# Shorter steps between a search and its expert, another share of filling, and narrower counting matmuls

## The chip, the cores and the metric

The kernel runs on 1 core of a Trainium2 chip. The metric is the time of one execution on the device in microseconds (us), the median of several runs. A profiled execution gives the rows below; its times count from the start of its span.

## The reference

Three layers in a row, on 4 sequences of 768 positions (3072 tokens of 512 features), all float32.

1. Banded attention, 8 heads of 64: each query sees the keys less than 16 positions away and the maxima of all 24 blocks of 32 keys (with the block means as values).
2. A first expert layer. The logits x @ w_gate of all tokens and 8 experts are sorted, and tokens are assigned greedily until an expert has CAP = 384 tokens. Then relu(x @ w1[e]) @ w2[e] for the tokens of each expert:

```
    for idx in order:
        tok, e = (int(idx) // E, int(idx) % E)
        if assigned[tok] >= 0 or counts[e] >= cap:
            continue
        assigned[tok] = e
```

3. A second expert layer with a skip score: out = x, and where x @ w_skip > 0, plus the gate weight times the chosen expert's two products.

## The kernel before

The work is written out by hand for each engine, and semaphores tie the engines together. It has four parts.

**Opening and attention.** 16 units (a sequence and a pair of heads), each of three groups of windows. SyncE's queue issues all loads in order. VectorE clears the borders of the key tiles `kc` and the gaps of `qz`, then the padded gates `wg1` and `wg2` (L941, L942), and signals `pads_ready`; TensorE runs seven matmuls on the padding as filling (L1404), then the scores of the first group (L1339, L1342). Behind attention, tiles of 128 token rows of its output are transposed on TensorE (`x_rows_tile`, L1399), copied out by ScalarE (L748) through four buffers and stored (L378). A buffer is written again only when its store has landed.

**Searches.** The greedy assignment closes one expert at a time, in 8 searches (`search(ph)` on VectorE, `window(w)` on TensorE). In each, V holds every token's best logit among the experts still open. It is transposed (L1547, L1548) into Vt, and 17 rounds look for the threshold bit by bit: VectorE counts how many values reach up to three candidates (L1028), TensorE adds the counts over partitions (CNT, L1557), VectorE picks the next candidates (L1043, L1045). A matmul spreads the threshold of each expert (TAU, L1567); VectorE takes the largest, `tau`, and the expert that has it (`oneE`, `e_f`, `e_i`). `e_i` lets SyncE load that expert's weights W1 and W2, 2 MB each (L381, L385). Then VectorE marks the tokens above `tau` and at it (GT), adds them up along the row (`scn`), and copies the row totals to `rowt` (L1072). Two matmuls turn these into offsets (BAS and BASN, L1571, L1572), and VectorE computes each token's `slot` (L1083). From that come one-hot tiles (`hot` L1092, `hot_blk` L1094, `hot_id` L314 and L315: on VectorE in search 0, on GpSimd in the others). TensorE folds them into a list (L1503), VectorE copies it (`folded`, L1000), TensorE unfolds it (L1511), and VectorE writes the token numbers `gidx` (L1006). GpSimd then gathers the rows of the expert's tokens in three tiles (L593), counted by one semaphore `xg_in`. Meanwhile VectorE takes the closed expert and the taken tokens out of the logits LM (L1099 to L1103) and forms the next V (L988 to L1015); the copies of `folded` and `gidx` stand between these steps.

**Products between the counts.** TensorE's list is fixed when the program is written. Expert k needs 3 transposes of rows (L1468), 32 products of the first layer (`product_1`, two instructions of 384 columns, L1479), 24 of the second (`product_2`, two instructions of 512 columns, L1493), and a tail for the second layer's gate. Each of these has a number of units: 3 for a first-layer product, 4 for a second-layer one, 2 for a transpose of rows. `room(w)` gives how many units may be placed in each of 22 gaps of window w: one before the rounds, 17 behind the counts, and four behind TAU, BAS, the fold and the lists. An item is placed when the running sum of units allows it whole. Window w carries the products of expert w - 1; window 0 has none, and TensorE runs filling matmuls there (`keep_busy`, L1540), as in the first two rounds of window 1. What is left runs behind search 7. TensorE keeps the order of its list: a wait holds all that stands behind it.

**Second layer.** Tiles of 128 tokens through layer1 (L1608) and layer2 (L1626), 4 MB of weights for each.

The count matmul reads `cnt` (8 columns) sixteen times over, so it has 128 columns; TAU, BAS and BASN have 128 columns too, of which 8, 2 and 1 are read.

## Time and profile before

| | |
|---|---|
| median of 3 runs | 844.89 us (843.51 to 848.12) |
| profiled execution | 842.21 us |
| its span | 840.4 us |
| TensorE matmuls busy | 800.1 us (95%) |
| VectorE busy | 465.7 us (55%) |
| ScalarE busy | 228.4 us (27%) |
| GpSimd busy | 216.2 us (26%) |

Attention ends at about 144 us of the span, search 0 at 194; the first product of the first expert layer starts at 203.60, and the last search's lists are read at about 544. From some 607 on the second layer runs. The 95% is a mean over stages: it does not say that TensorE is the limit in each. Matmuls are pipelined and the ends are modelled, so the distance from one start to the next says more than a busy time.

### The profile page before, as it was taken

To read this page: it belongs to the slowest core of one execution; us is meant where nothing else is said; L and a number is where in the kernel's file an instruction comes from. 1 tells how busy PE (TensorE), PEld (TensorE's weight loads), DVE (VectorE), ACT (ScalarE), POOL (GpSimd) and SP (SyncE) were. 2 spreads that over 40 slices of the span, in tenths; PEclk is the share of its full clock that TensorE was granted. 3 is DMA by queue.
4 is the path that set the end of the run, shared out by engine and by line. 5 is a ranking of instruction groups with operands and counts; after the bars stand their busy time and mean duration, and the time that the engine had idled before them with its cause. 6 is when DMAs were issued, how large, how long until landed. Compare 5 with 4: busy or idle time off the path is not lost.

```text
span 840.4 us, 15143 instructions
## 1 busy us (share of the span) xinstructions
PE 800.1 (95%) x5002; PEld 512.0 (61%) x5002; DVE 465.7 (55%) x2153; ACT 228.4 (27%) x681; POOL 216.2 (26%) x313
## 2 busy tenths in 40 slices
PE   7999998897899999999999999999999999999996
PEld 6878786785445455454544545455577686777762
DVE  7989896777777676776766677507049100000000
ACT  6888786501103121120211212121111111110101
POOL 7888883001030120302112030120300321111110
PEclk9999999999999999999999999999999999999999
DMA  9967650625070531706225071436988999898983
GB/s 272 294 226 220 205 144 21 266 69 186 0 284 30 190 123 25 264 25 236 77 102 186 26 265 48 166 147 257 356 313 312 414 350 346 309 344 305 331 322 114
DMA packets 64505, 171.66 MB, mean 204 GB/s; under 512 B 5584, under 2 KB 5584, under 8 KB 64448
## 3 DMA queue, kind: packets, MB, share of 16 engines
q1 hardware_dynamic: 54512, 143.70, 48.5%
q0 software_dynamic: 6480, 20.91, 6.9%
q10 hardware_dynamic: 3456, 6.29, 1.9%
q8 instruction: 36, 0.59, 0.3%
q14 instruction: 21, 0.17, 0.1%
HBM read 148.41 MB, written 22.81 MB: 204 GB/s over the span
## 4 chain that ended last, share of the span: by engine, by line
PE 74%; DVE 13%; DMA 5%; issue 3%; POOL 2%; SPq 1%; ACT 1%; DVEq 0%; POOLq 0%; ACTq 0%
PE bank L1493 17%; PE bank L1479 16%; PE bank L1626 11%; PE bank L1608 11%; DVE junk L1028 5%; PE bank L1342 3%; PE bank L1369 3%; PE bank L1351 2%; DMA kc<-in_kT 2%; PE bank L1557 2%; DMA weights<-in_moe_w 1%; PE bank L1468 1%; PE bank L1684 1%; PE bank L1339 1%; PE bank L1652 1%
## 5 line engine op out<-in xcount | busy, mean ns | idle before, releaser
L1479 PE MATMUL bank<-features,weights 128*128 128x384 f32 x512 | 182.3, 497 | 0.6 <-ACT features L753 0.6
L1493 PE MATMUL bank<-weights 128*128 128x512 f32 x384 | 179.2, 602 | 0.0
L1028 DVE TENSOR_SCALAR_CACHE_REDUCE junk<-Vt,cand 128x192 bf16<-128x192 f32 x376 | 136.1, 409 | 4.8
L1479 PEld LDWEIGHTS bank<-features,weights 128*128 128x128 f32 x512 | 89.5, 191 | 50.6 <-issue 5.6
L1608 PEld LDWEIGHTS bank<-x2T,weights 128*128 128x128 f32 x896 | 102.2, 192 | 5.9 <-issue 5.9
L1608 PE MATMUL bank<-x2T,weights 128*128 128x128 f32 x896 | 102.6, 275 | 0.0
L1493 PEld LDWEIGHTS bank<-weights 128*128 128x128 f32 x384 | 66.8, 190 | 58.4 <-issue 56.5
L1626 PE MATMUL bank<-weights,h2T 128*128 128x512 f32 x224 | 98.8, 593 | 0.4 <-ACT h2T L820 0.4
L1188 DVE SCALAR_TENSOR_TENSOR o<-bank,gate,x 128x512 f32<-128x512 f32 x14 | 10.5, 751 | 155.0 <-PE bank L1626 155.0
L758 ACT ACTIVATE weights<-bank 128x384 f32<-128x384 f32 x64 | 31.4, 491 | 141.3 <-PE bank L1479 141.3
L1626 PEld LDWEIGHTS bank<-weights,h2T 128*128 128x128 f32 x224 | 41.3, 190 | 46.5 <-issue 46.5
L702 ACT ACTIVATE pr<-bank,nmx 128x120 f32<-128x120 f32 x192 | 67.0, 374 | 5.1 <-DVE nmx L899 4.9
L820 ACT ACTIVATE h2T<-bank 128x512 f32<-128x512 f32 x28 | 16.6, 597 | 161.9 <-PE bank L1608 161.9
L314 POOL TENSOR_TENSOR hot_id<-hot,pnum 128x384 bf16<-128x384 f32 x7 | 8.2, 1168 | 180.2 <-DVE hot L1092 180.2
L1342 PEld LDWEIGHTS bank<-kw,qz 128*128 128x128 f32 x384 | 51.5, 195 | 1.0
L503 POOL TENSOR_TENSOR pr<-pr,rinv 128x480 f32<-128x480 f32 x48 | 47.3, 986 | 15.7 <-DVE rinv L905 14.1
L1342 PE MATMUL bank<-kw,qz 128*128 128x120 f32 x384 | 51.2, 277 | 0.0
L1043 DVE TENSOR_SCALAR_CACHE_REDUCE reached<-bank 128x7 f32<-128x7 f32 x120 | 19.9, 166 | 54.5 <-PE bank L1557 54.5
L762 ACT ACTIVATE weights<-bank 128x512 f32<-128x512 f32 x24 | 14.3, 598 | 126.9 <-PE bank L1493 126.9
L1557 PEld LDWEIGHTS bank<-cnt,same_e 128*128 128x128 bf16 x136 | 13.1, 96 | 57.2 <-DVE junk L1028 53.7
L593 POOL DMA_INDIRECT weights<-x_rows,gidx x24 | 23.6, 985 | 89.6 <-DVE gidx L1006 59.5
L600 POOL DMA_INDIRECT out<-weights,tok_i x24 | 23.7, 986 | 85.1 <-ACT weights L762 82.2
(333 smaller groups left out, 1056.7 us busy)
## 6 DMA issues: line engine op xcount, KB each, us to landing
weights<-in_moe_w SPq DMA_DIRECT2D x52, 2048.0 KB, 9.9
vw<-in_vwin SPq DMA_DIRECT2D x16, 576.0 KB, 5.1
qc<-in_qT SPq DMA_DIRECT2D x16, 384.0 KB, 5.6
kc<-in_kT SPq DMA_DIRECT2D x16, 384.0 KB, 6.1
vc<-in_vT SPq DMA_DIRECT2D x16, 384.0 KB, 7.4
x_rows<-xr SPq DMA_DIRECT2D x24, 256.0 KB, 2.3
y_rows<-weights ACTq DMA_DIRECT2D x24, 256.0 KB, 2.0
weights<-x_rows,gidx POOLq DMA_INDIRECT x24, 3.7
```

Of the source, the lines that this page charges most:

```text
L503: g.tensor_tensor(pr[:, n % NP, :, :], pr[:, n % NP, :, :], rinv[:, n % NP, :].unsqueeze(2).to_broadcast([128, GW, KW]), ALU.mult) \
L600: g.indirect_dma_start(out=out, out_offset=bass.IndirectOffsetOnAxis(ap=tok_i[:, j:j + 1], axis=0), in_=yb[:, j, :], in_offset=None).then_ ...
L702: ins = a.activation(pr[:, n % NP, w, :], SC[n % 3][:, KW * w:KW * w + KW], ACT.Exp, scale=SCALE, bias=nmx[:, n % NP, w:w + 1], accum_out= ...
L758: a.activation(hT[:, r, :], HB[r % 2][:, 0:CAP], ACT.Relu).then_inc(s["h_act"], 1)
L1028: ins = ve.tensor_scalar(junk[:, c, :], Vt[:, :], cand[:, c:c + 1].bitcast(fp32), 0.0, ALU.is_ge, ALU.add, accum_out=cnt[:, c:c + 1])
L1342: ins = mm(SC[n % 3][:, KW * w:KW * w + KW], qz[u % 2][:, GW * gr + w, :], kw[u % 2][:, GW * gr + w, :], start=False, stop=(w == GW - 1))
L1369: ins = mm(OB[n % 2][D * j:D * j + D, QW * w:QW * w + QW], vw[i][:, GW * gr + w, D * j:D * j + D], pT[:, n % 2, 128 * w + QW * j:128 * w + ...
L1479: ins = mm(HB[r % 2][:, 0:CAP], w1[:, c, 128 * r:128 * r + 128], xgT[:, c, :], start=(c == 0), stop=(c == KC - 1))
L1493: ins = mm(YB[j % 2][:, :], hT[:, r, 128 * j:128 * j + 128], w2[:, r, :], start=(r == 0), stop=(r == FC - 1))
L1557: mm(CNT, same_e[:, :], cnt[:, :].unsqueeze(1).to_broadcast([128, WIDE // 8, 8]), start=True, stop=True).then_inc(s["cnt_mm"], 1)
L1608: ins = mm(HB2[h][:, 128 * c:128 * c + 128], W1[:, buf, k * F + at:k * F + at + 128], x2T[par][:, k, :], start=(k == 0), stop=(k == KC - 1))
L1626: ins = mm(YB2[par][:, :], h2T[:, f, :], W2[:, buf, f * DM:f * DM + DM], start=(f == 0), stop=(f == FC - 1))
```

## The change

In VectorE's chain behind the threshold, comparisons and products are joined in one instruction, the expert number is computed behind the row totals, and the two base matmuls add up in PSUM, so that their result is read as a pointer scalar without copies. `oneE` is finished later, ahead of the update of LM. In search 0's list `folded` and `gidx` are copied earlier (`first_list`). CNT, TAU and BAS become as narrow as what is read. The gathered tiles have a semaphore each, and TensorE, SyncE and GpSimd wait for these; on GpSimd and SyncE all three are waited for where `xg_in` was. Two row tiles instead of four stand ahead of window 0, the others move two later. `room()` changes for windows 1 and 2, and the filling changes in window 0, in the first rounds of window 1, and at the opening, where the gate padding is cleared first.

```diff
-    WIDE = 128
...
-        diag = sb("diag", [E, WIDE])
+        diag = sb("diag", [E, E])
...
-        rowt = sb("rowt", [128, WIDE], bf16)
-        base = sb("base", [128, 4])
+        rowt = sb("rowt", [128, 3], bf16)
+        rank = sb("rank", [128, 2, NT])
...
-        VTP, CNT, TAU = SM[:, 0:256], SM[:, 256:256 + WIDE], SM[:, 384:384 + WIDE]
-        BAS, BASN, FOLD, IDS = SM[:, 0:WIDE], SM[:, WIDE:2 * WIDE], SM[0:2 * SB, 384:384 + SLOTS // SB], SM[:, 448:448 + CT]
+        VTP, CNT, TAU = SM[:, 0:256], SM[:, 256:264], SM[:, 384:384 + E]
+        BAS, FOLD, IDS = SM[:, 0:2], SM[0:2 * SB, 384:384 + SLOTS // SB], SM[:, 448:448 + CT]
...
-                        .then_inc(s["xg_in"], 16)
+                        .then_inc(s[f"xg_in{j}"], 16)
...
+            ve.memset(wg1[:, :, :], 0.0)
+            ve.memset(wg2[:, :, :], 0.0).then_inc(s["pads_ready"], 1)
             for i in range(NB):
                 ve.memset(kc[i][:, 0:BAND], 0.0)
...
-            ve.memset(wg1[:, :, :], 0.0)
-            ve.memset(wg2[:, :, :], 0.0).then_inc(s["pads_ready"], 1)
             block_maxima(0)
...
                 o.step(ve.tensor_reduce(m, src, X, ALU.max))
+                first_list = isinstance(ids_of, int) and ids_of == 0
+                if first_list:
+                    fold_out(ids_of)
                 o.step(ve.tensor_tensor(tmp, src, bc(m, shape, 2), ALU.is_equal))
-                if ids_of is not None:
+                if first_list:
+                    ids_out(ids_of)
+                elif ids_of is not None:
                     fold_out(ids_of)
...
-                if ids_of is not None:
+                if ids_of is not None and not first_list:
                     ids_out(ids_of)
...
-                o.step(ve.tensor_reduce(tau[:, :], TAU[:, 0:E], X, ALU.max))
-                o.step(ve.tensor_scalar(oneE[:, :], TAU[:, 0:E], tau[:, :], None, ALU.is_equal))
-                o.step(ve.tensor_tensor(oneE[:, :], oneE[:, :], revE[:, :], ALU.mult))
+                o.step(ve.tensor_reduce(tau[:, :], TAU, X, ALU.max))
+                o.step(ve.scalar_tensor_tensor(out=oneE[:, :], in0=TAU, scalar=tau[:, :], in1=revE[:, :],
+                                               op0=ALU.is_equal, op1=ALU.mult))
                 o.step(ve.tensor_reduce(oneM[:, :], oneE[:, :], X, ALU.max))
-                o.step(ve.tensor_scalar(oneE[:, :], oneE[:, :], oneM[:, :], None, ALU.is_equal))
+                o.step(ve.scalar_tensor_tensor(out=t1[:, :, :], in0=bc(oneE[:, :], full, 1), scalar=oneM[:, :], in1=V[:, :, :],
+                                               op0=ALU.is_equal, op1=ALU.mult))
+                o.step(ve.tensor_reduce(mx[:, :], t1[:, :, :], X, ALU.add))
+
+                o.step(ve.tensor_scalar(GT[:, 0, :], mx[:, :], tau[:, :], None, ALU.is_gt))
+                o.step(ve.tensor_scalar(GT[:, 1, :], mx[:, :], tau[:, :], None, ALU.is_equal))
+                for h in range(2):
+                    o.step(ve.tensor_tensor_scan(scn[:, h, :], GT[:, h, :], zero1[:, :], 0.0, ALU.add, ALU.add))
+                ve.tensor_copy(rowt[:, 1:3], scn[:, :, NT - 1]).then_inc(s["rows_ready"], 1)
+                o.step(ve.scalar_tensor_tensor(out=rank[:, :, :], in0=scn[:, :, :], scalar=float(-BIG_SLOT), in1=GT[:, :, :],
+                                               op0=ALU.add, op1=ALU.subtract))
                 o.step(ve.tensor_scalar(e_f[:, :], oneM[:, :], -1.0, float(E), ALU.mult, ALU.add))
                 if not isinstance(ph, int) or ph > 0:
                     dve.wait_ge(s["expert_read"], ph)
                 ve.tensor_copy(e_i[:, :], e_f[:, :]).then_inc(s["expert_ready"], 1)
-                o.step(ve.tensor_tensor(t1[:, :, :], V[:, :, :], bc(oneE[:, :], full, 1), ALU.mult))
...
-                dve.wait_ge(s["base_mm"], ph + 1)
-                o.step(ve.tensor_copy(base[:, 0:2], BAS[:, 0:2]))
-                o.step(ve.tensor_copy(base[:, 2:3], BASN[:, 0:1]))
-                o.step(ve.tensor_tensor(base[:, 1:2], base[:, 1:2], base[:, 2:3], ALU.add))
+                dve.wait_ge(s["base_mm"], ph + 1)
                 for h in range(2):
-
-                    o.step(ve.scalar_tensor_tensor(out=scn[:, h, :], in0=scn[:, h, :], scalar=base[:, h:h + 1],
-                                                   in1=GT[:, h, :], op0=ALU.add, op1=ALU.subtract))
-                    o.step(ve.scalar_tensor_tensor(out=scn[:, h, :], in0=scn[:, h, :], scalar=float(-BIG_SLOT),
+                    o.step(ve.scalar_tensor_tensor(out=rank[:, h, :], in0=rank[:, h, :], scalar=BAS[:, h:h + 1],
                                                    in1=GT[:, h, :], op0=ALU.add, op1=ALU.mult))
...
                 o.step(ve.tensor_scalar(sel[:, :], slot[:, :], CAP - 0.5, None, ALU.is_lt))
-
+                o.step(ve.tensor_scalar(oneE[:, :], oneE[:, :], oneM[:, :], None, ALU.is_equal))
...
-            for _ in range(7):
+            for _ in range(11):
                 mm(LG[0:32, 0:128], wg2[:, 0, :], wg2[:, :, :].rearrange("p c e -> p (c e)"), start=True, stop=True)
...
-            for t in range(4):
+            for t in range(2):
                 x_rows_tile(t)
...
                 if w == 1:
-                    return [0] + [0, 0, 6] + [6] * (ROUNDS - 3) + [15, 28, 4, 8]
-                return [8] + [9, 8] * 7 + [9] * 3 + [15, 28, 4, 4 if w == 2 else 8]
+                    return [0] + [0, 6] + [6, 9, 6, 6] * 3 + [6, 9, 6] + [13, 22, 4, 8]
+                if w == 2:
+                    return [8] + [9, 8] * 7 + [8] * 3 + [13, 22, 4, 4]
+                return [8] + [9, 8] * 7 + [9] * 3 + [15, 28, 4, 8]

             def load_x(k, j):
-                if j == 0:
-                    pe.wait_ge(s["xg_in"], 16 * CT * (k + 1))
-
+                pe.wait_ge(s[f"xg_in{j}"], 16 * (k + 1))
...
-                keep_busy(w, 3)
+                keep_busy(w, 4)
...
                 if w == 0:
-                    x_rows_tile(4)
-                    x_rows_tile(5)
+                    x_rows_tile(2)
+                    x_rows_tile(3)
+                if w == 1:
+                    keep_busy(0, 5)
                 keep_busy(w, 2)
...
-                    mm(CNT, same_e[:, :], cnt[:, :].unsqueeze(1).to_broadcast([128, WIDE // 8, 8]),
-                       start=True, stop=True).then_inc(s["cnt_mm"], 1)
-                    if w == 0 and n < NT // 2 - 3:
-                        x_rows_tile(2 * n + 6)
-                        x_rows_tile(2 * n + 7)
-                    keep_busy(w, 3 if n < NT // 2 - 3 else 6)
-                    if w == 1 and n < 2:
-                        keep_busy(0, 6)
+                    mm(CNT, same_e[:, :], cnt[:, :], start=True, stop=True).then_inc(s["cnt_mm"], 1)
+                    if w == 0 and n < NT // 2 - 2:
+                        x_rows_tile(2 * n + 4)
+                        x_rows_tile(2 * n + 5)
+                    keep_busy(w, 3 if n < NT // 2 - 2 else 6)
+                    if w == 1 and n == 0:
+                        keep_busy(0, 7)
...
-                keep_busy(w, 14)
+                keep_busy(w, 11)
...
-                mm(BAS, tri[:, :], rowt[:, :], start=True, stop=True)
-                mm(BASN, ones_bf[:, :], rowt[:, :], start=True, stop=True).then_inc(s["base_mm"], 1)
-                keep_busy(w, 22)
+                mm(BAS, tri[:, :], rowt[:, 1:3], start=True, stop=False)
+                mm(BAS, ones_bf[:, :], rowt[:, 0:2], start=False, stop=True).then_inc(s["base_mm"], 1)
+                keep_busy(w, 17)
...
-                keep_busy(w, 2)
+                keep_busy(w, 1)
                 ids(w)
-                keep_busy(w, 5)
+                keep_busy(w, 9)
```

## Rows read from the trace of the kernel before

**Rows 1.** Busy time by stretch: busy us (instructions) of each engine, granted clock, DMA share, GB/s.

```profile
196.00:252.00 56.00, 49.40 (x199) 24.60 (x200) 40.98 (x238) 6.81 (x13) 8.85 (x11) 1.00 0.45 157
...
302.45:353.04 50.59, 50.02 (x218) 25.72 (x217) 35.91 (x204) 9.61 (x19) 8.40 (x11) 1.00 0.36 130
```

**Rows 2.** Chain of waits in the opening: start us, us, what.

```profile
9.02 15.14 DMA kc<-in_kT
```

**Rows 3.** Timeline of the opening: start, us, engine, line, operation, count, [idle before it].

```profile
3.23 3.20 PE L1404 MATMUL bank<-wg 128*32 128x128 f32 x14 [3.23 <-DVE wg L942]
...
7.05 1.90 PE L1342 MATMUL bank<-kw,qz 128*128 128x120 f32 x8
...
9.47 1.05 PE L1342 MATMUL bank<-kw,qz 128*128 128x120 f32 x8
```

**Rows 4.** Timeline around the start of search 0 and its fifteenth count.

```profile
145.77 0.21 DVE L934 TENSOR_TENSOR V<-LM,t 128x48 f32<-128x48 f32 x1
...
146.85 0.27 PE L1547 MATMUL bank<-ident,V 128*128 128x128 f32 x1
...
150.54 0.65 PE L1399 MATMUL bank<-ident,xT 128*128 128x128 f32 x4 [1.17 <-ACT xr L748]
...
153.59 0.23 PE L1557 MATMUL bank<-cnt,same_e 128*128 128x128 bf16 x1
...
176.45 0.23 PE L1557 MATMUL bank<-cnt,same_e 128*128 128x128 bf16 x1 [0.28 <-DVE junk L1028]
```

**Rows 5.** Two matmul lines: duration ns min/median/max, first and last start, form.

```profile
L1557 PE MATMUL bank<-cnt,same_e x136: 219/219/230, 148.7 to 530.3; 128*128 128x128 bf16 x136
...
L1511 PE MATMUL bank<-folded,unfold x64: 161/162/174, 192.5 to 544.4; 32*128 32x3 bf16 x64
```

**Rows 6.** Timeline of VectorE in the tail of search 0.

```profile
181.88 0.17 DVE L1056 TENSOR_REDUCE tau<-bank 128x1 f32<-128x8 f32 x1 [1.20 <-PE bank L1567]
...
185.06 0.17 DVE L1072 CAST rowt<-scn 128x2 bf16<-128x2 f32 x1
...
187.18 0.18 DVE L1083 SCALAR_TENSOR_TENSOR slot<-scn 128x24 f32<-128x24 f32 x1
...
193.48 0.16 DVE L1006 CAST gidx<-bank 128x3 int32<-128x3 f32 x1
```

**Rows 7.** Chain of waits up to the first product.

```profile
196.83 4.04 DMA weights<-x_rows,gidx
...
202.26 0.67 PE bank L1468 x4
...
203.60 0.59 PE bank L1479
```

**Rows 8.** Timeline, the queue of SyncE: the first expert's weights.

```profile
184.42 0.43 SPq L381 DMA_DIRECT2D weights<-in_moe_w  x1
```

**Rows 9.** Timeline of TensorE in the tail of search 2.

```profile
279.49 0.48 PE L1567 MATMUL bank<-diag,ones 8*128 8x128 f32 x2
279.91 2.85 PE L1479 MATMUL bank<-features,weights 128*128 128x384 f32 x8
283.43 0.23 PE L1571 MATMUL bank<-rowt,tri 128*128 128x128 bf16 x1 [0.67 <-DVE rowt L1072]
...
283.55 6.23 PE L1493 MATMUL bank<-weights 128*128 128x512 f32 x14
289.71 0.77 PE L1503 MATMUL bank<-hot_blk,hot_id 128*32 128x24 bf16 x24
...
293.45 0.33 PE L1547 MATMUL bank<-ident,V 128*128 128x128 f32 x1 [0.58 <-DVE V L1015]
```

**Rows 10.** Timeline of TensorE in search 3.

```profile
323.87 0.23 PE L1557 MATMUL bank<-cnt,same_e 128*128 128x128 bf16 x1 [0.24 <-DVE junk L1028]
323.93 2.15 PE L1479 MATMUL bank<-features,weights 128*128 128x384 f32 x6
325.92 0.22 PE L1557 MATMUL bank<-cnt,same_e 128*128 128x128 bf16 x1
```

More of the change, by code:

```diff
@@ L262, in banded_attention_two_moe_layers @@
             onehot_ready blk_ready id_mm idp_ready ids_ready tok_c
[L263 removed]
+            xg_in0 xg_in1 xg_in2 xg_tr xgT_ready w_in0 w_in1 w_in2 w_in3 w2_in0 w2_in1 w2_in2 w2_in3 w1_lanes w2_lanes h_mm h_act y_mm y_evac y_tr yT_ready l2_mm l2T_ready l2_tr l2_evac y_out y_st y_written
             gate_sub gate_exp rows8_ready base8_mm teA_ready onehot2_ready id2_mm gid2_ready route2_ready
@@ L383, in load_weights @@
                 if rows_first:
-                    sp.wait_ge(s["xg_in"], 16 * CT)
+                    for j in range(CT):
+                        sp.wait_ge(s[f"xg_in{j}"], 16)
                 sp.dma_start(W2[:, 2 * par, :].rearrange("p (c f) -> p c f", c=FC),
@@ L612, in _ @@
             keep_ids(0)
-            pool.wait_ge(s["xg_in"], 16 * CT)
+            for j in range(CT):
+                pool.wait_ge(s[f"xg_in{j}"], 16)
             with pool.Fori(1, E) as ph:
@@ L619, in _ @@
                 keep_ids(ph)
-                wait(pool, "xg_in", 16 * CT * (ph + 1))
+                for j in range(CT):
+                    wait(pool, f"xg_in{j}", 16 * (ph + 1))
                 o.leave(E)
@@ L1071, in search @@
                     o.step(ve.tensor_tensor_scan(scn[:, h, :], GT[:, h, :], zero1[:, :], 0.0, ALU.add, ALU.add))
-                ve.tensor_copy(rowt[:, 0:2], scn[:, :, NT - 1]).then_inc(s["rows_ready"], 1)
+                ve.tensor_copy(rowt[:, 1:3], scn[:, :, NT - 1]).then_inc(s["rows_ready"], 1)
+                o.step(ve.scalar_tensor_tensor(out=rank[:, :, :], in0=scn[:, :, :], scalar=float(-BIG_SLOT), in1=GT[:, :, :],
+                                               op0=ALU.add, op1=ALU.subtract))
+                o.step(ve.tensor_scalar(e_f[:, :], oneM[:, :], -1.0, float(E), ALU.mult, ALU.add))
+                if not isinstance(ph, int) or ph > 0:
+                    dve.wait_ge(s["expert_read"], ph)
+                ve.tensor_copy(e_i[:, :], e_f[:, :]).then_inc(s["expert_ready"], 1)
                 dve.wait_ge(s["base_mm"], ph + 1)
-                o.step(ve.tensor_copy(base[:, 0:2], BAS[:, 0:2]))
-                o.step(ve.tensor_copy(base[:, 2:3], BASN[:, 0:1]))
-                o.step(ve.tensor_tensor(base[:, 1:2], base[:, 1:2], base[:, 2:3], ALU.add))
                 for h in range(2):
-                    o.step(ve.scalar_tensor_tensor(out=scn[:, h, :], in0=scn[:, h, :], scalar=base[:, h:h + 1],
-                                                   in1=GT[:, h, :], op0=ALU.add, op1=ALU.subtract))
-                    o.step(ve.scalar_tensor_tensor(out=scn[:, h, :], in0=scn[:, h, :], scalar=float(-BIG_SLOT),
+                    o.step(ve.scalar_tensor_tensor(out=rank[:, h, :], in0=rank[:, h, :], scalar=BAS[:, h:h + 1],
                                                    in1=GT[:, h, :], op0=ALU.add, op1=ALU.mult))
-                o.step(ve.scalar_tensor_tensor(out=slot[:, :], in0=scn[:, 0, :], scalar=float(BIG_SLOT),
-                                               in1=scn[:, 1, :], op0=ALU.add, op1=ALU.add))
+                o.step(ve.scalar_tensor_tensor(out=slot[:, :], in0=rank[:, 0, :], scalar=float(BIG_SLOT),
+                                               in1=rank[:, 1, :], op0=ALU.add, op1=ALU.add))
                 if not isinstance(ph, int) or ph > 0:
```

7 lines of the change are left out of this document (1 added, 6 removed).

## The prediction

> **What bounds the kernel now.** I read the busy times by stretch first. From the third search on, TensorE is busy for 50.02 of 50.59 us, in six stretches alike, at a granted clock of 1.00: there an edit pays only if it shortens TensorE's own list or an idle gap. In the stretch that holds search 1 it is busy for 49.40 of 56.00 us [rows 1]; search 0, ahead of it, has no product to cover it at all. The chain of waits is read next: in the opening it hangs on a load of kc that takes 15.14 us and lands at 24.16 [rows 2]. The timelines then show, for search 0, a chain that alternates between VectorE and one small matmul [rows 4, 6], the row gather behind it [rows 7], and in the later windows which instruction ends a gap [rows 9, 10].
>
> I sum against the profiled execution, 842.21 us (span 840.4 and 1.8 around it). The median of the runs is 844.89, 2.7 above it; I subtract the same gain from the median.
>
> **Opening.** The padding memsets go ahead of the other memsets, so filling starts some 1.8 us earlier (before: at 3.23) with 22 matmuls instead of 14. The eight score matmuls that started at 7.05 took 1.90 us, the next eight 1.05 [rows 3]: the first were still at the lower of TensorE's two clock levels, 1.2 GHz, and the earlier filling may save up to 0.9 there. I count 0: the kc load behind it was issued by a queue that never waited, and its landing [rows 2] holds VectorE's next maxima whatever TensorE does. Bounds: -0.3 (zeros written later) to 0.9.
>
> **Search 0, up to the last count.** V is done at 145.98, but its transposes start at 146.85, since tiles 2 and 3 and the filling stand ahead [rows 4]. With two tiles and four fills ahead, TensorE is free at about 145.6 and starts at 146.05: 0.8 sooner. Then tile 7 waited 1.17 us for ScalarE [rows 4], which waited for the stores of the first tiles; the third count came at 153.59. The stores land as before, but tiles run two later in the list: tile 6 goes at 150.5, tile 7 at 151.15, its six fills end at 152.25, and the third count starts at 152.3, 1.3 sooner (0.8 of them the start, 0.5 the smaller stall). From there a round takes 22.86/12 = 1.905 us [rows 4], VectorE's turn. A count matmul lasts 219 ns with 128 columns and one with 3 columns lasts 162 [rows 5]: 0.45 ns a column, so 8 columns give 165, and 0.053 less a round. Thirteen rounds: 0.7. The threshold matmul comes 2.0 sooner; itself it goes from 128 to 8 columns in two passes, each 0.107 less streaming: 0.2. VectorE starts on tau 2.2 sooner.
>
> **Search 0, from tau to the first product.** From tau to the row totals took 3.18 us (181.88 to 185.06) [rows 6]. Two narrow steps merge or go, and e_f and e_i move behind: four steps at about 0.18, as narrow ones last there; the wide step takes a pointer scalar (+0.07, bound 0 to 0.15): 0.64 less. From totals to slot took 2.12 us [rows 6]: two copies, an add and two steps of the four before the last go; rank, e_f and e_i run while TensorE sums, and the totals land at about +0.5, rank and its followers end at +0.55. Two pointer steps of 0.27 follow: 1.1 in all, 1.0 less. From slot to gidx took 6.30; oneE now adds 0.26, but the fold is copied one step and gidx three steps sooner (0.39 each, less 0.15 of waiting for the second matmul group): 0.7 less. gidx comes 2.2 + 0.64 + 1.0 + 0.7 = 4.5 us sooner, at 189.0. V of search 1, which pays oneE and the wait, comes 3.3 sooner (190.95 for 194.2).
> The third gather thus lands at 196.4 for 200.87. Before, TensorE then took two transposes, a wait for ScalarE and a third, 2.73 us to the first product [rows 7]; with a semaphore for each tile only the third is left, 202.26 to 203.60 in the same chain, 1.35. The product can start at 197.8 for 203.6. The weights don't stop it: e_i moves behind 1.7 us of other work, so they are issued at 184.0 for 184.42 [rows 8], and 8.0 us to landing gives 192.
>
> **Window 1.** Unit counts from room() and the list give the items per round; a first-layer product costs 1.99/3 = 0.665 [rows 10], a second-layer one 6.16/7 = 0.88 [rows 9], a count 0.055. Rows go in round 1 instead of 2, and its third transpose waits for the gather (196.45), so the third count is at 197.0; products start behind it. Four of the later rounds hold three products (2.05 us), nine hold two (VectorE's 1.85). The last count falls at 223.7 for 227.1: 3.4 sooner, with 18 units (4.0 us) more done. Behind it stands one second-layer product instead of two first-layer ones, 0.45 less ahead of the threshold. TensorE's gap ahead of the row totals in this tail and in that of search 2 (0.67 there [rows 9]) shrinks by 0.6. At the transposes for search 2 the kernel is 5.6 us early and 10 units (2.6 us) ahead in work: 8.2 gained.
>
> **Window 2.** It carries 2.6 us less work, so that lead is spent on time. Its tail is planned too short: from row totals to transposes TensorE has 7.2 us of items for a chain that took 10.0 (283.43 to 293.45, with 0.58 idle [rows 9]) and will take 9.3. That is 1.0 more idle than before; four short rounds add 0.2, the row-total gap gives back 0.85, the threshold 0.2: 0.2 lost.
>
> **Windows 3 to 7.** Their allowances are unchanged, but the sum up to search 2 is 349 units for 350, so whole items fall differently: four rounds instead of two hold only 1.31 to 1.33 us of work. Such a round costs what VectorE needs: 0.24 idle is shown, 1.805 - 1.365 = 0.44 from start to start [rows 10]; after, 0.39. The tally gives 1.81 us of idle in the rounds for 0.95. Against it go the gaps at totals, fold, lists and transposes, 0.5, and the threshold and base matmuls, 0.24: the first took 0.42 from its start to the next [rows 9] and becomes about 0.2. Net 0.1 lost a window, 0.8 with the change of phase. Nothing behind search 7 moves by itself.
>
> **Does a narrow count free TensorE?** Ahead of the next product 0.06 us passed after a 128-column count [rows 10]. I leave it: the next weights are 128 columns of f32 and load behind it. The other bound is the fold, 24 columns with narrow weights: (0.77 - 0.17)/23 = 0.026 [rows 9]. Between 0.055 and 0.026 I take the first, the row of this very pair.
> The Trainium skill (TensorE: Matmul & The Clock Gate, "Back-to-back issue gap") puts matmuls of 1 to 64 columns at a floor near 25 ns; by it the counts would shrink so, and the second rival would be the forecast.
>
> Sum: 8.2 - 0.2 - 0.8 = 7.2 us; my round-by-round tally, which puts the old windows at 50.08 for 50.59, gives 7.1. 842.21 - 7.1 = 835.1 profiled, 844.9 - 7.1 = 837.8 as the median.
>
> **Rivals.**
> Narrow counts pay on TensorE: 0.029 in some 95 counts that stand between products, 2.7 more, 835.1. For it: the fold's pace; against: its weights are 32 columns of bf16.
> The gain is partly given back in the steady windows: the items shifted between rounds include transposes that wait on ScalarE. Each further 0.5 a window costs 2.5, gain 4.6, 840.3. For it: two more short rounds are certain; against: order within the list is the same.
> The gather wait takes the place of the mended chain: the row transposes now stand a round earlier, ahead of count 2, so a late gather holds the search in full. If the gathers, issued from 189.5, queue behind the weights until 192 and lose 4 us, the gain is 3.1, 841.8. Against: the weights' traffic ends about a microsecond before their landing.
> Slower: TensorE's clock. The 128-column counts were padding; narrower, with two tiles less ahead, they could let the level fall to 1.2 GHz in the rounds of search 0 or window 1. A round with six fills then takes 2.7 for 1.85, one with two products 2.77: 0.9 each. From the eighth such round the gain of 7.1 is gone; fifteen rounds cost 13.5, giving 851.3. Against: in window 1 the rounds were no denser than 1.39 of 1.905, and the clock stood at 1.00 [rows 1].
> The Trainium skill (same page, "The HAM clock gate") has the clock follow how busy TensorE was lately; that speaks for this rival, and the trace bears it out only in the opening.
>
> **How the numbers follow.** Forecast 0.66 (own range 835 to 841, from the bounds above and the runs' scatter), narrow counts pay 0.10, given back 0.12, gather 0.07, clock 0.05. A measurement tells about 0.5% from no change, 4.2 us, so faster means below 840.7. Nearly all of the forecast, all of the narrow counts, half of the third and a third of the fourth case: 0.79 faster; 0.16 within; the clock 0.05 slower. Range 833.5 to 842.5: it takes in four cases.
>
> **What would show it.** Right: the first transposes of V near 146.05; rounds of 1.85 in search 0; tau to row totals 2.5 and totals to slot 1.1; the first product near 197.8; short rounds four a window from search 3 on, with periods of 50.5 to 50.9; kc still on the chain at 24. Wrong: a period below 50.2 (narrow counts pay), a level of 0.50 in the slices, a gap ahead of the third count of window 1 of more than 0.6, or a start of V's chain that has moved with the opening.

## The result, and the profile after

The changed kernel takes 839.61 us (median of 6 runs, 838.37 to 841.90) beside 846.29 for the kernel before on the same chip: a ratio of 0.9938 with a 95% interval of 0.9913 to 0.9963. It is faster by 0.6%, 5.2 us on the 844.89 shown; the interval reaches from 3.1 to 7.4 us. (The quotient of the two medians is 0.9921, inside this interval.) Forecast were 7.1 us less (837.8, range 833.5 to 842.5): right within its range, with a size missed by 1.9 us, which the interval alone would not tell from a hit; the trace below shows where it was lost. The profiled execution took 839.7 us, its span 837.9.

The chain of waits (start, us, what) still hangs on kc in the opening, and it landed later than before [rows 2], at 25.94 for 24.16:

```profile
10.03 15.91 DMA kc<-in_kT
```

All that follows has this 1.8 us on it: attention ends at 145.69 for 143.90. Below, "from attention" counts from the first transpose of a row tile behind attention (L1402), which takes that difference out. Of the timeline (start, us, engine, line, what, count, [idle before it]) these are the lines of search 0 and its tail that answer to [rows 4, 6, 7]:

```profile
145.69 1.04 PE L1402 MATMUL bank<-ident,xT 128*128 128x128 f32 x8
...
147.91 0.33 PE L1550 MATMUL bank<-ident,V 128*128 128x128 f32 x1 [0.28 <-DVEq L1018]
...
153.43 0.18 PE L1562 MATMUL bank<-cnt,same_e 128*128 128x8 bf16 x1
...
167.82 0.66 PE L1402 MATMUL bank<-ident,xT 128*128 128x128 f32 x4 [0.72 <-ACT xr L750]
...
181.68 0.17 DVE L1063 TENSOR_REDUCE tau<-bank 128x1 f32<-128x8 f32 x1 [1.15 <-PE bank L1571]
...
184.21 0.17 DVE L1075 CAST rowt<-scn 128x2 bf16<-128x2 f32 x1
...
185.33 0.18 DVE L1086 SCALAR_TENSOR_TENSOR slot<-rank 128x24 f32<-128x24 f32 x1
...
190.95 0.16 DVE L1013 CAST gidx<-bank 128x3 int32<-128x3 f32 x1 [0.26 <-PE bank L1514]
...
198.24 0.63 PE L1471 MATMUL bank<-ident,weights 128*128 128x128 f32 x4 [0.34 <-ACT features L755]
...
199.56 1.56 PE L1482 MATMUL bank<-features,weights 128*128 128x384 f32 x4 [0.68 <-ACT features L755]
```

Tau to row totals is 2.53 us (3.18 before), totals to slot 1.12 (2.12), slot to gidx 5.62 (6.30). The first product is 53.87 us behind the end of attention, for 59.70 (203.60 - 143.90): 5.83 sooner. The early stall on ScalarE (1.17 behind the first count in [rows 4]) is gone, and one of 0.72 has come nine rounds later, behind the tenth count.

Busy time by stretch, for windows 1 to 4 (window w is the stretch from the transposes of V for search w to the next; us, then busy us and instructions of PE, PEld, DVE, ACT, POOL, then granted clock, DMA share, GB/s); to be read beside [rows 1]:

```profile
193.12:239.55 46.43, 42.29 (x181) 22.04 (x182) 35.00 (x198) 6.20 (x12) 4.09 (x6) 1.00 0.34 112
239.55:287.67 48.12, 46.40 (x209) 24.38 (x208) 35.11 (x198) 9.60 (x19) 8.22 (x10) 1.00 0.38 142
287.67:338.77 51.10, 50.16 (x216) 25.75 (x217) 35.10 (x198) 9.60 (x19) 8.62 (x11) 1.00 0.37 136
338.77:389.87 51.10, 50.16 (x217) 25.71 (x216) 35.12 (x198) 9.60 (x19) 8.26 (x11) 1.00 0.34 125
```

The last two rows are the finding. Their windows are 51.10 long where those of before were 50.59, and TensorE idles 0.94 of it for 0.57. The gain up there is partly spent again, window by window. From the end of attention to the second layer the kernel needs 458.87 us for 463.74: 4.87 less, and with the late landing 3.08 less in the trace. The second layer takes 0.6 more in this execution (233.38 for 232.78).

The timeline of TensorE in window 4 shows where (three of its rounds, then the tail):

```profile
348.86 0.18 PE L1562 MATMUL bank<-cnt,same_e 128*128 128x8 bf16 x1 [0.24 <-DVE junk L1035]
...
352.90 0.18 PE L1562 MATMUL bank<-cnt,same_e 128*128 128x8 bf16 x1 [0.19 <-DVE junk L1035]
...
368.09 0.17 PE L1562 MATMUL bank<-cnt,same_e 128*128 128x8 bf16 x1
368.12 2.18 PE L1482 MATMUL bank<-features,weights 128*128 128x384 f32 x6
370.14 0.17 PE L1562 MATMUL bank<-cnt,same_e 128*128 128x8 bf16 x1
...
376.37 0.38 PE L1571 MATMUL bank<-diag,ones 8*128 8x8 f32 x2
376.69 3.49 PE L1482 MATMUL bank<-features,weights 128*128 128x384 f32 x10
380.02 0.17 PE L1575 MATMUL bank<-rowt,tri 128*128 128x2 bf16 x1
```

Short rounds end in a wait for VectorE; there are four in this window (the other two, at 357.40 and 361.66, idle 0.23 and 0.20). In window 4 of the kernel before two rounds end so, 0.24 each. A full round still takes 2.05 (368.09 to 370.14), as in [rows 10]. The threshold pair (the two instructions of TAU) passes in 0.32 (376.37 to 376.69) for 0.42 [rows 9].

### The profile page after: what moved, and what is told of

Read it like the earlier page. It is cut to its first block, busy times and chain, and to the rows that moved or that the text cites. A ratio compares the mean times of both kernels' runs of the same rounds, so it can differ in the third digit from the quotient of the medians.

```text
span 837.9 us, 15121 instructions
## 1 busy us (share of the span) xinstructions
PE 800.1 (95%) x4996; PEld 512.7 (61%) x4996; DVE 460.3 (55%) x2113; ACT 228.3 (27%) x681; POOL 214.9 (26%) x313
## 4 chain that ended last, share of the span: by engine, by line
PE 76%; DVE 12%; DMA 5%; issue 2%; POOL 2%; SPq 1%; ACT 1%; DVEq 0%; POOLq 0%; ACTq 0%
PE bank L1496 19%; PE bank L1482 16%; PE bank L1630 12%; PE bank L1612 11%; DVE junk L1035 6%; PE bank L1345 3%; PE bank L1372 3%; PE bank L1354 2%; DMA kc<-in_kT 2%; PE bank L1562 1%; DMA weights<-in_moe_w 1%; PE bank L1688 1%; DVE reached L1050 1%; DVE cand L1052 1%; PE bank L1342 1%
```

## The experiments

Eleven kernels were run. "Steady windows" are the means of windows 3 to 6, from one transpose of V to the next. All ratios are to the kernel before, run on the same chip, with 95% intervals. The single rows are of one profiled execution of each kernel. "From attention" is used as above.

**One unit of work more** (the changed kernel, window 2's last round 9 instead of 8):

```diff
-                    return [8] + [9, 8] * 7 + [8] * 3 + [13, 22, 4, 4]
+                    return [8] + [9, 8] * 7 + [8, 8, 9] + [13, 22, 4, 4]
```

> The changed kernel with one unit more in window 2 (its last round 9 instead of 8), so that the sum up to search 2 is 350 as before. Theory A (the shifted items cost the steady windows): from window 3 on the rounds hold the items of the kernel before, with two short rounds instead of four; the period of 51.1 us falls to 50.15 (50.6 less the 0.44 that the narrower threshold and the shorter chain gave), five windows give 4.5 to 5 us, so 10 to 12 us faster than the kernel before. Rival B (the narrow matmuls or the semaphores make the steady windows longer): the period stays near 51.1, no gain over the changed kernel.

Measured: 836.53 us, 0.9902 (0.9873 to 0.9931), beside 0.9938 for the change. Steady windows take 49.97 for 51.10. Busy by stretch, windows 3 and 4:

```profile
286.86:336.88 50.02, 49.61 (x217) 25.94 (x217) 35.17 (x198) 9.61 (x19) 8.67 (x11) 1.00 0.38 139
336.88:386.84 49.96, 49.55 (x218) 25.88 (x216) 35.16 (x198) 9.61 (x19) 8.27 (x11) 1.00 0.36 131
```

Idle is 0.41 where it was 0.94; the busy time, whose ends are modelled, is 0.6 less as well. The timeline of TensorE in window 4 has two short rounds again, for four:

```profile
346.92 0.18 PE L1562 MATMUL bank<-cnt,same_e 128*128 128x8 bf16 x1 [0.22 <-DVE junk L1035]
...
367.06 0.18 PE L1562 MATMUL bank<-cnt,same_e 128*128 128x8 bf16 x1 [0.19 <-DVE junk L1035]
```

One unit in one place shifts which whole items fall into each later round, in every window behind it: 1.13 us a window, all of it between the first count and the last (32.35 for 33.48). Theory A holds. Of its 10 to 12 us the trace has 10.7 from attention to the second layer (453.00 for 463.73); the runs give 8.3, with an interval of 5.8 to 10.7.

**The opening as before** (padding cleared behind attention's memsets, 7 filling matmuls):

```diff
+            ve.memset(wg1[:, :, :], 0.0)
+            ve.memset(wg2[:, :, :], 0.0).then_inc(s["pads_ready"], 1)
             block_maxima(0)
...
-            for _ in range(11):
+            for _ in range(7):
```

> The changed kernel with the old opening: padding cleared late, seven filling matmuls. Theory A (the level that fell back to 1.2 GHz at about 9 us is what made attention end 1.8 us late): attention ends near 143.9 again, 1.5 to 2 us faster than the changed kernel. Rival B (the kc load landed late by itself, the loads scatter from run to run): no difference beyond 0.5 us in the medians, attention ends anywhere between 143.9 and 145.7.

Measured: 840.62 us, 0.9950 (0.9924 to 0.9976), so no gain that the runs can tell from the 0.9938 of the change, and theory A's 1.5 to 2 us did not come. Attention ends at 144.07, but the gather of the first expert's rows then came late in this execution. Timeline of TensorE in window 1:

```profile
194.59 1.07 PE L1471 MATMUL bank<-ident,weights 128*128 128x128 f32 x8
197.33 0.66 PE L1471 MATMUL bank<-ident,weights 128*128 128x128 f32 x4 [1.67 <-DMA weights<-x_rows,gidx]
197.82 0.17 PE L1562 MATMUL bank<-cnt,same_e 128*128 128x8 bf16 x1
198.67 2.93 PE L1482 MATMUL bank<-features,weights 128*128 128x384 f32 x4 [0.68 <-ACT features L755]
201.39 0.21 PE L1562 MATMUL bank<-cnt,same_e 128*128 128x8 bf16 x1
```

and busy by stretch around it:

```profile
194.90:198.40 3.50, 1.42 (x12) 1.00 (x10) 1.67 (x13) 1.47 (x3) 0.00 (x0) 1.00 0.03 9
198.40:202.00 3.60, 3.33 (x6) 1.88 (x7) 1.50 (x11) 0.22 (x1) 0.00 (x0) 0.53 0.87 242
202.00:206.00 4.00, 3.72 (x14) 1.87 (x13) 2.92 (x20) 0.49 (x1) 0.00 (x0) 1.00 0.80 306
```

TensorE was busy for 1.42 of 3.50 us; then the granted clock is 0.53 for a stretch, near the lower level of 1.2 GHz, and four product instructions take 2.93 us for the 1.56 of the changed kernel's. Window 1 is 49.37 long for 46.43. Of these 2.9 us, 1.35 stand ahead of the first product (7.79 from the transposes of V for 6.44), which is the late gather; nearly all the rest lies in the stretch at the lower level. This is the slower rival in small, behind the late-gather rival.

**The allowances as before** (`room()` of the kernel before in all windows, all else changed):

```diff
-                if w == 2:
-                    return [8] + [9, 8] * 7 + [8] * 3 + [13, 22, 4, 4]
-                return [8] + [9, 8] * 7 + [9] * 3 + [15, 28, 4, 8]
+                return [8] + [9, 8] * 7 + [9] * 3 + [15, 28, 4, 4 if w == 2 else 8]
```

> The changed kernel with room() of the kernel before in all windows (filling as changed, so round 1 of window 1 is empty on TensorE). Theory A (units moved into window 1 make about half of the gain): first product and search 0 as changed, window 1 keeps idle rounds, but windows 3 to 7 at 50.15; about 2.6 lost in window 1 and 4.5 gained later, so 1 to 3 us faster than the changed kernel. Rival B (the allowances are worth more than the phase costs): slower than the changed kernel by 2 us or more.

Measured: 835.10 us, 0.9890 (0.9863 to 0.9916). Steady windows 49.97, window 1 46.54 and window 2 48.94 for the change's 46.43 and 48.12. The new allowances are worth 0.9 us in windows 1 and 2 and lose 1.13 in every window behind. The old ones are the better; the new ones with their unit back do as well. Theory A named the direction but a smaller size: 4 us faster than the changed kernel by the two ratios, for 1 to 3.

**Only the narrow matmuls** (the kernel before with CNT, TAU, BAS and BASN 8, 8, 2 and 2 columns wide):

```diff
-                    mm(CNT, same_e[:, :], cnt[:, :].unsqueeze(1).to_broadcast([128, WIDE // 8, 8]),
+                    mm(CNT, same_e[:, :], cnt[:, :],
```

> The kernel before with only the counting, threshold and base matmuls as narrow as what is read (8, 8 and 2 columns). Theory A (a narrow count shortens VectorE's wait by 0.05 and frees nothing on TensorE): rounds of 1.855 in search 0 and 1, the steady period shorter by 0.1 to 0.3; 1.5 to 3 us faster than before. Rival B (it frees TensorE, 0.03 a count): 4 us or more. Rival C (it costs the steady windows): period above 50.6, no gain.

Measured: 843.55 us, 0.9984 (0.9960 to 1.0008): no difference that the runs can tell, and less than the 1.5 to 3 us of theory A, which the interval does not exclude. In the trace, rounds of search 0 take 1.855 for 1.905; steady windows 50.25 for 50.60, of which the rounds give 0.17, the threshold 0.10, the rest 0.08. Timeline of TensorE in search 3, to be held against [rows 10]:

```profile
323.64 0.17 PE L1557 MATMUL bank<-cnt,same_e 128*128 128x8 bf16 x1
323.67 2.18 PE L1479 MATMUL bank<-features,weights 128*128 128x384 f32 x6
325.69 0.17 PE L1557 MATMUL bank<-cnt,same_e 128*128 128x8 bf16 x1
```

2.05 from count to count, both times. The next product starts 0.03 behind the narrow count instead of 0.06, and the round is not shorter for it.

The profiled execution, at 844.83 one of the longer ones, is no measure of what the narrow matmuls are worth. Up to the transposes for search 7 it is 3.25 us ahead of the kernel before (348.68 from attention for 351.93). Then all of it goes: the last copy of GpSimd waits 3.93 us for the scattered rows to land, where it waited 2.02, so TensorE stands idle until VectorE has the totals that the second layer's routing needs, and the granted clock is 0.50 behind it. Timeline of TensorE:

```profile
567.55 0.19 PE L1584 MATMUL bank<-row,tri 128*128 128x8 bf16 x1 [3.22 <-DVE row L1199]
567.60 0.17 PE L1585 MATMUL bank<-row,ones_bf 128*128 128x8 bf16 x1
567.62 2.91 PE L1479 MATMUL bank<-features,weights 128*128 128x384 f32 x4
```

Before, the idle time there was 1.31 and the same four instructions took 1.54. Whether the landing is late by chance or by the change isn't shown.

**Only the opening** (the kernel before with the changed one):

```diff
-            for _ in range(7):
+            for _ in range(11):
```

> The kernel before with nothing but the new opening: the two padding memsets ahead of the others on VectorE, and 11 fill matmuls there instead of 7. Theory A (the opening of the change costs time: the load of kc is issued a microsecond later, at 10.0 for 9.0, and lands later, so attention is late): attention ends at 144.9 to 145.7 for 143.9, and the kernel is 1 to 1.8 us slower, 846 to 847 us beside 845. Theory B (what was seen in the changed kernel is scatter of the DMA, and a single fall of the clock that comes anywhere): the end of attention stays within 0.3 us, and so does the time.

Measured: 844.58 us, 0.9979 (0.9964 to 0.9993). No loss, so theory A falls, though attention ended 0.96 later in this profile than before, outside the 0.3 of theory B. Over the thirteen profiles, attention ends at 143.66, 143.90, 144.07, 144.57, 145.38, 147.05, 147.63 and 148.13 with the old opening and at 144.63, 144.86, 145.11, 145.69 and 149.33 with the new: the spread inside each group is wider than the 1.8 us between the two kernels. The chain of waits of an execution with the old opening (the kernel of the unit and the old opening, below) shows such a late one:

```profile
8.09 1.94 SPq L338
10.07 17.77 DMA kc<-in_kT
```

It lands at 27.84, with the opening whose landing in [rows 2] is 24.16.

**Wide counts in the changed kernel** (CNT 128 columns again, threshold and base narrow):

```diff
-                    mm(CNT, same_e[:, :], cnt[:, :], start=True, stop=True).then_inc(s["cnt_mm"], 1)
+                    mm(CNT, same_e[:, :], cnt[:, :].unsqueeze(1).to_broadcast([128, 16, 8]), start=True, stop=True).then_inc(s["cnt_mm"], 1)
```

> The changed kernel with the counting matmuls 128 columns wide again, all else as changed (threshold, base and fold narrow). Theory A (the narrow count shortens a round that is short of filling by its duration, 0.05 to 0.07 us, and frees nothing of TensorE): rounds of search 0 take 1.90 for 1.84 us, window 0 grows by 0.8, steady rounds together by at most 0.2 a window; 2 us slower than changed, 841 to 842 us. Theory B (narrow counts also free TensorE time in filled rounds, 0.05 in each of the 17): steady windows grow by 0.85, all in all 7 us, 846 us.

Measured: 841.54 us, 0.9962 (0.9939 to 0.9984). Rounds of search 0 take 1.905, steady windows 51.31 for 51.10 (the rounds 33.68 for 33.48). Theory A, in all its numbers but window 0 (0.2 longer for 0.8), whose missing part is hidden by a smaller stall on the row tiles in this execution (its one long round took 2.06, for 2.55).

**Narrow matmuls and the changed chain** (plan, fills, row tiles, semaphore and opening of before). The core of the edit:

```diff
-                o.step(ve.tensor_scalar(oneE[:, :], TAU[:, 0:E], tau[:, :], None, ALU.is_equal))
-                o.step(ve.tensor_tensor(oneE[:, :], oneE[:, :], revE[:, :], ALU.mult))
+                o.step(ve.scalar_tensor_tensor(out=oneE[:, :], in0=TAU, scalar=tau[:, :], in1=revE[:, :],
+                                               op0=ALU.is_equal, op1=ALU.mult))
...
-                mm(BASN, ones_bf[:, :], rowt[:, :], start=True, stop=True).then_inc(s["base_mm"], 1)
+                mm(BAS, ones_bf[:, :], rowt[:, 0:2], start=False, stop=True).then_inc(s["base_mm"], 1)
```

> The kernel before with the narrow matmuls and with the changed chain of VectorE between threshold, totals, slots and row indices (with the second base matmul accumulated into the first); the plan of work, the fills, the row tiles' order, the gathers' semaphore and the opening stay as before. Theory A (the chain's gains count in every window, since the waits at totals and list end sooner while TensorE has too little work there): steady windows 49.97 for the 50.25 of the narrow kernel, window 0 44.6 to 45 for 46.3, time 839 to 841. Theory B (the chain's gain in steady windows is swallowed by the filled rounds, and only window 0 gains): steady windows stay at 50.25, time 841.5 to 842.5.

Measured: 839.14 us, 0.9938 (0.9912 to 0.9964), for 0.9984 without the chain; the intervals just touch. In the traces, up to the transposes for search 7, the chain is worth 3.12 us (345.56 from attention for 348.68) and the narrow matmuls ahead of it 3.25, so neither is shown to be the larger part. Window 4 takes 49.97 for 50.25; 0.19 of it lies between threshold and row totals. Window 2, whose tail is planned shorter, takes 48.94 for 50.25, with 0.65 less ahead of the row totals and 0.66 less ahead of the transposes. Theory A holds there. Window 3 stays at 50.61, since its row transposes wait 0.86 for the gathers here. Search 0 gained nothing in length, against the 1.3 to 1.7 us expected: window 0 is 46.71 for 46.33. Its first round took 0.45 more in this execution (3.23 for 2.78), and its tail is only 0.08 shorter, for it is held by filling. Timeline of TensorE in it:

```profile
184.80 2.96 PE L1542 MATMUL bank<-ident 128*128 128x128 f32 x25
187.59 0.17 PE L1573 MATMUL bank<-rowt,tri 128*128 128x2 bf16 x1
...
187.64 5.16 PE L1542 MATMUL bank<-ident 128*128 128x128 f32 x44
192.73 0.77 PE L1505 MATMUL bank<-hot_blk,hot_id 128*32 128x24 bf16 x24
```

Neither matmul group has waited: the 14 and 22 fills of before last longer than the shortened chain. Threshold to row totals takes 3.54 and on to the fold 5.14; with the change's 11 and 17 fills 3.18 and 4.32. Behind search 7 this profile too has a late landing and a fall of the clock (TensorE's wait at the same place is 2.95), 2.8 us in all.

**The unit and the old opening together** (the changed kernel with both edits above):

```diff
-            for _ in range(11):
+            for _ in range(7):
...
-                    return [8] + [9, 8] * 7 + [8] * 3 + [13, 22, 4, 4]
+                    return [8] + [9, 8] * 7 + [8, 8, 9] + [13, 22, 4, 4]
```

> The changed kernel with two things mended: one unit of work more in the last round of window 2, so that the windows' 350 units are whole again, and the opening as before. Theory A (both faults add up: 3.1 us for the unit, 1 to 1.6 for the opening): 834.5 to 835.5 us, attention ends at 144.0, steady windows take 49.97. Theory B (with the earlier end of attention the gather of the first rows is what the first product waits for, so the opening's gain is lost there): 836 to 837 us, a wait on the weights or x rows of over 1 us ahead of the first product.

Measured: 835.39 us, 0.9892 (0.9852 to 0.9932), steady windows 49.98. The time is theory A's, its reason is not: attention ended at 147.63 here, and the interval doesn't tell the time from that of the unit alone (0.9902).

**The list more closely filled in window 2** (the last kernel with 8 and 7 units behind fold and list, for 4 and 4):

```diff
-                    return [8] + [9, 8] * 7 + [8, 8, 9] + [13, 22, 4, 4]
+                    return [8] + [9, 8] * 7 + [8, 8, 9] + [13, 22, 8, 7]
```

> The changed kernel with the opening as before, one unit more in the last round of window 2 (350 whole again), and in window 2's tail 8 and 7 units instead of 4 and 4 behind fold and list: two second-layer products more where TensorE waited 0.51 us ahead of the list and 0.54 ahead of the transposes. Theory A (these are real holes and later windows keep their 209 units, so what is done earlier is missing at the end): window 2 grows from 48.1 to 48.4, the end of layer 1 comes 1.75 us of work sooner, net 1.3 to 1.5 us less than without it: 833.5 to 834.5. Theory B (TensorE overshoots the chain of VectorE there, and the search pays the whole of the products): window 2 takes 49.9, time 835.4 as without.

Measured: 835.72 us, 0.9883 (0.9846 to 0.9919). Window 2 is 48.56 for 48.13, and from search 7 to the second layer 109.69 for 111.36. Windows 3 to 6 lose 0.43 in between, nearly all in window 6 (50.45 for 49.97), where the row transposes now wait 0.33 for their gather. Net 0.8 us: theory A's direction, less than its 1.3 to 1.5. The time does not show it. Its runs stand in two groups (832.41 to 833.32, and 838.12 to 838.73); the profiled one is of the upper, and in it the first gather was late by 1.7 us, the clock fell behind it, and window 1 took 49.46.

**Products wait for all gathers** (the unit and old opening, one wait for three tiles as before):

```diff
-                pe.wait_ge(s[f"xg_in{j}"], 16 * (k + 1))
+                if j == 0:
+                    for i in range(CT):
+                        pe.wait_ge(s[f"xg_in{i}"], 16 * (k + 1))
```

> The changed kernel with the opening as before and the whole 350 units, but with the row transposes of an expert waiting for all three gathers, not for their own. Theory A (waiting for one's own tile takes two transposes and ScalarE's copies off the way to the first product): from the transposes of V of search 1 to the first product 8.0 to 8.3 us for 6.43, count 3 of search 1 comes 1.4 later, window 1 grows by 1 to 1.5 us or carries that much less; time 836.5 to 837. Theory B (in window 1 the rounds take it back, since VectorE sets their pace): first product later by 1.5, window 1 and the time within 0.3 us of the kernel without this edit, 835.4.

Measured: 839.93 us, 0.9938 (0.9917 to 0.9960), for 0.9892: more than either theory. Window 1 is 47.48 for 46.42, and window 2 50.11 for 48.13. Timeline of TensorE in window 2:

```profile
245.89 1.96 PE L1498 MATMUL bank<-weights 128*128 128x512 f32 x4
249.65 0.52 PE L1473 MATMUL bank<-ident,weights 128*128 128x128 f32 x3 [1.80 <-DMA weights<-x_rows,gidx]
```

Window 3 is 50.76 for 50.02 as well. So the semaphore for each tile carries 3.8 us here (1.06, 1.98 and 0.74), not only the first product. The likely reason is that a list that is further ahead meets the next expert's rows sooner; it fits that with the allowances of before window 2 takes 48.94 with either semaphore (the chain kernel above and the one with the allowances as before).

**Chain and row tiles** (narrow matmuls, chain, and the row tiles as changed):

```diff
-            for t in range(4):
+            for t in range(2):
                 x_rows_tile(t)
```

> The kernel before with narrow matmuls, the changed chain of VectorE, and now also the x row tiles and their filling in search 0 as changed (two tiles instead of four ahead of the transposes of V, one fill more there, tiles two rounds later). Opening, plan of window 1 and 2 and gathers' semaphore as before. Theory A (fewer tiles ahead bring the transposes forward, and the stall on the copies of tile 7 shrinks): transposes 2.22 us after attention for 2.94, from count 1 to count 3 3.6 us for 5.1; 2 us less than the kernel without it, about 837. Theory B (the stores of x rows, not the order of the tiles, set the stall, so it only moves): transposes 0.72 sooner but a round later in search 0 longer by 0.7 or more; 838.5 to 839.

Measured: 836.61 us, 0.9911 (0.9882 to 0.9940), for 0.9938. The transposes come 2.22 behind attention for 2.94, counts 1 to 3 take 3.61 for 5.08, and a round of 2.66 stands later: of 2.2 us, 0.8 moved. Both theories had a part: the transposes for search 1 stand 1.34 sooner from attention (48.31 for 49.65). But window 1 gives 1.06 of it back (47.52 for 46.46). Timeline of TensorE in it:

```profile
199.49 1.09 PE L1470 MATMUL bank<-ident,weights 128*128 128x128 f32 x8 [0.90 <-DMA weights<-x_rows,gidx]
```

The kernel without the new order did not wait there, and at the transposes for search 7 the two are level (345.49 and 345.56 from attention). The intervals of the runs overlap too. So the order of the tiles shortens search 0, and that the whole kernel gains by it isn't shown.

## Why the prediction was right, and where it was short

- **Opening, counted 0.** Right, and the new opening alone is no slower. The trace's 1.8 us later landing lies inside the scatter of the thirteen profiles.
- **Search 0 to the last count.** Transposes 2.22 us from attention (forecast 2.15); the third count 7.74 (forecast 8.4); rounds 1.855 (forecast 1.85). The stall was not only smaller, part of it moved to the tenth round.
- **Tau to first product.** 2.53, 1.12 and 5.62 for 2.54, 1.12 and 5.6; gidx at 45.26 from attention for 45.1, the first product at 53.87 for 53.9. The weights did not stop it (landed at 193.78). That fewer fills are needed for these gains went unsaid in the sum; the kernel with the chain and the old filling shows it.
- **Windows 1 and 2.** At the transposes for search 2 the kernel is 5.15 early from attention (forecast 5.6). The 0.4 was missing already at those for search 1, 2.92 early for 3.3. Window 2 gives 2.42 (forecast 2.4). The lead in these windows holds only with a semaphore for each tile, of which the sum priced just the first product: in the kernel with the unit and the old opening, one wait for all makes windows 1 to 3 longer by 3.8.
- **Windows 3 to 7: the mis-sized term.** Forecast was 0.1 lost a window, 0.8 in all; measured are 0.50 in each of four and 0.68 up to the second layer: 2.7. The four short rounds came as said: the rounds grew by 0.95 (forecast 0.86). What should pay for it was put too high: 0.74 in the sum, 0.44 in the trace (threshold to totals 0.28, totals to fold 0.05, fold to list 0.11, list to transposes 0). By the kernels with single edits, 0.18 of it is the narrow threshold and base (forecast 0.24) and 0.27 the shorter gaps (forecast 0.5). [Rows 9] are of search 2, whose tail is planned shorter; the 0.58 idle there does not stand in the steady windows, where the list ahead of the transposes is full.
- **The threshold pair, 0.10 for 0.20.** The distance to the next product went from 0.42 to 0.32: one 0.107, not two. The narrow base made up part of it: its pair passes in 0.05 for 0.12.
- **A narrow count frees nothing on TensorE.** Right: 2.05 a full round at either width; wide counts put back only 0.20 a window, in the short rounds.
- **The rivals.** The second (given back in the steady windows) took place at about its stated size, 0.4 more a window than the sum, 1.9 in all. Its mechanism did not: no transpose waits on ScalarE in window 4, and the loss is the short rounds of the forecast with less to pay for them. The measured 839.61 lies nearer to this rival's 840.3 than to the forecast. The late gather and the lower clock came together in two of the profiles, at 3 us each, not in the changed kernel's own window 1. Narrow counts did not pay on TensorE.

Sum from attention: 5.15 + 2.42 - 2.7 = 4.87, and 5.2 by the runs. With one unit more it is 8.3. What a unit does had been seen in the count of short rounds, but was priced against gains that the same windows did not have. The round-by-round tally had put the old windows at 50.08 for a measured 50.59; that half microsecond, as large as the loss in question, was on the table and was not followed up.

What stays open: the late first gather, by 1.7 us in 2 of the 7 profiles in which each tile has its own semaphore, what brings the late landing of kc, and the late landing behind search 7 in two profiles, were not traced to a cause. The new filling counts were not run by themselves.

## What to carry to other kernels

Where whole items are placed by a running sum, a change of the sum by one unit shifts every later gap: list the items by round for each of the steady windows and count the rounds that come out shorter than the partner's turn, before looking at the window that was edited. A chain between engines that is made shorter needs its filler made shorter too, and each gap that pays for a loss must be read in the very window in which the loss is counted. Waiting for one's own part of a transfer gained most here where the list ran ahead. A single trace of an execution is split into stretches before it is used to price an edit: late landings and a lower clock, 3 us in several of these profiles, are as large as the edits.

## What the runs showed of the hardware

- Duration by width: the count takes 219 ns with 128 columns and 169 with 8 (162 with 3 in the unfold), yet the time from count to count in a full round stays at 2.05 us. Here the duration is latency to whoever waits for the count, and no time of the products.
- The granted clock falls to 0.50 for single short stretches, in other places from run to run: among others, within the first 20 us in three of the thirteen profiles, in window 1 in three, between search 7 and the second layer in two; in five profiles it does not fall again until the last microseconds. Busy by stretch in the opening of the changed kernel:

```profile
5.60:9.10 3.50, 1.65 (x12) 1.18 (x10) 3.39 (x9) 0.28 (x1) 2.73 (x7) 1.00 0.97 334
9.10:12.50 3.40, 3.26 (x14) 2.72 (x15) 2.10 (x4) 2.58 (x9) 1.64 (x2) 0.50 1.02 228
```

  Filling from 1.25 on raised the level early (the first scores took 1.05 us for the 1.90 of [rows 3]), and TensorE then stood idle for 0.94 and 1.05 us in between; the next scores were at the lower level. What was saved on the first eight was paid on the next, in this execution; in two others with the same opening (the allowances as before, and the opening alone) both groups took 1.05 and the level stayed at 1.00. The Trainium skill (TensorE: Matmul & The Clock Gate, "The HAM clock gate") has the clock follow how busy the engine was lately; the trace agrees, with 1.65 busy of 3.50 us ahead of this fall and 1.42 of 3.50 ahead of the one in window 1. Little activity does not bring a fall each time, though: the kernel with the chain and the row tiles stays at 1.00 behind a stretch that is busy for 1.07 of 3.50. Busy by stretch:

```profile
191.30:194.80 3.50, 1.07 (x9) 0.61 (x8) 2.63 (x10) 0.00 (x0) 2.89 (x3) 1.00 0.53 163
194.80:198.80 4.00, 3.42 (x27) 2.96 (x27) 3.07 (x20) 0.00 (x0) 0.48 (x3) 1.00 0.40 118
```

- One such fall in window 1, together with the late gather ahead of it, cost 2.9 us (49.37 for 46.43), more than most edits of this study are worth. Another in window 1, in the kernel with only narrow matmuls, fell on filling ahead of a gather that had not landed: TensorE still waited 0.16 us for it, so this fall cost next to nothing there.
- Time and mean granted clock go together from execution to execution. Of the kernel before, beside the first four experiments, the five executions at a mean of 0.999 took 842.7 to 845.1 us, the four at 0.994 or less 845.8 to 849.4 (a single one of 4565 us, at 1.000, is left out).
